# A DRAIN on GpSimd in each pass of the loop over expert tiles

## What is computed

```python
def _moe2_ref(x, w_gate, w_local, w1, w2):
    logits = np.einsum('bsd,de->bse', x, w_gate)
    local_gate = 1.0 / (1.0 + np.exp(-np.einsum('bsd,de->bse', x, w_local).squeeze(-1)))
    for b in range(B):
        prev_e = -1
        for s in range(S):
            fresh_e = int(np.argmax(logits[b, s]))
            if s == 0 or local_gate[b, s] < 0.5:
                e = fresh_e
            else:
                e = prev_e if prev_e >= 0 else fresh_e
            prev_e = e
            ...                                  # p: softmax of logits[b, s]
            h = np.maximum(x[b, s] @ w1[e], 0.0)
            out[b, s] = p[e] * (h @ w2[e])
```

## Time and profile before

| | |
|---|---|
| median of 3 runs | 627.32 us (628.27, 627.32, 627.22) |
| profiled execution, its own time | 628.33 us |
| its span, first to last instruction | 626.3 us |
| mean granted TensorE clock | 0.995 |
| busy: PE, DVE, ACT, POOL | 97%, 66%, 51%, 28% of the span |

### The profile page before, as it was taken

How to read it: one execution, slowest core, us unless ns; L and a number is a source line. 1 busy time by engine, 2 the same in 40 slices (tenths; PEclk the granted TensorE clock), 3 DMA queues, 4 the chain that set the end, 5 groups by cost and what they waited for, 6 DMA issues and landing times.

```text
span 626.3 us, 14701 instructions
## 1 busy us (share of the span) xinstructions
PE 607.7 (97%) x4483; PEld 504.6 (81%) x4484; DVE 410.8 (66%) x1164; ACT 321.3 (51%) x698; POOL 176.2 (28%) x241
## 2 busy tenths in 40 slices
PE   7999999999999999999999999999999999999994
PEld 6778888888788888889979877788788888888883
DVE  3767779745779697786979959948626336372621
ACT  5767779667515714631544853647516226351610
POOL 4545545600000000000000231675723412552240
PEclk9999999999999999999999999999999999999998
DMA  8987786002210010000004751787825414672000
GB/s 302 374 269 249 265 278 220 18 2 85 74 62 0 1 50 18 0 33 35 0 32 155 247 223 57 282 304 258 326 82 174 167 39 131 214 245 93 12 29 3
DMA packets 32935, 84.66 MB, mean 135 GB/s; under 512 B 4602, under 2 KB 7418, under 8 KB 32896
## 3 DMA queue, kind: packets, MB, share of 16 engines
q1 hardware_dynamic: 26816, 70.03, 32.0%
q0 software_dynamic: 3200, 8.92, 4.2%
q10 hardware_dynamic: 2880, 5.24, 2.6%
HBM read 76.04 MB, written 9.70 MB: 137 GB/s over the span
## 4 chain that ended last, share of the span: by engine, by line
PE 82%; DVE 8%; issue 3%; ACT 2%; POOL 2%; DMA 1%; POOLq 0%; DVEq 0%; ACTq 0%
PE banks L884 21%; PE banks L886 20%; PE banks L885 20%; PE banks L755 3%; PE banks L1074 3%; PE banks L822 2%; DVE we_lo L1526 2%; PE banks L831 2%; PE banks L785 2%; PE banks L769 1%; PE banks L993 1%; PE banks L799 1%; PE banks L795 1%; DMA xg<-x_rows,rows_in 1%; PE banks L846 1%
## 5 line engine op out<-in xcount | busy, mean ns | idle before, releaser
L1493 DVE CUSTOM_DVE_ANT_0 product<-x,xT 128x512 f32<-128x512 f32 x120 | 77.9, 688 | 0.5 <-DMA xT<-in_w 0.3
L1790 ACT ACTIVATE prob<-neg,negmax 128x160 f32<-128x160 f32 (+1 forms) x136 | 59.1, 436 | 30.3 <-DVE negmax L1204 20.6
L1768 DVE TENSOR_SCALAR hid<-banks 128x512 f32<-128x512 f32 x34 | 23.5, 691 | 72.4 <-PE banks L886 71.2
L1900 ACT ACTIVATE k_sum<-banks 128x512 f32<-128x512 f32 (+2 forms) x40 | 21.3, 534 | 90.9 <-PE banks L886 86.3
L884 PE MATMUL banks<-we_hi,hid_hi 128*128 (+1 forms) x160 | 66.4, 415 | 0.2 <-DVE hid_lo L1601 0.2
L884 PE MATMUL banks<-we_hi,xg_hi 128*128 (+1 forms) x160 | 64.6, 404 | 0.6 <-issue 0.6
L686 POOL MEMSET xg<- 128x1024 f32 x1 | 1.0, 952 | 220.9 <-ACT k_raw L1893 220.9
L886 PE MATMUL banks<-we_hi,xg_lo 128*128 (+1 forms) x160 | 62.6, 391 | 0.0
L885 PE MATMUL banks<-we_lo,hid_hi 128*128 (+1 forms) x160 | 62.6, 391 | 0.0
L886 PE MATMUL banks<-we_hi,hid_lo 128*128 (+1 forms) x160 | 62.6, 391 | 0.0
L885 PE MATMUL banks<-we_lo,xg_hi 128*128 (+1 forms) x160 | 62.4, 390 | 0.0
(11 more groups left out here) (295 smaller groups left out, 1486.0 us busy)
## 6 DMA issues: line engine op xcount, KB each, us to landing
xT<-in_w_e SPq DMA_DIRECT2D x36, 512.0 KB, 4.3
raw_end<-in_w_e SPq DMA_DIRECT2D x36, 512.0 KB, 5.0
qk<-in_qk_t SPq DMA_DIRECT2D x32, 448.0 KB, 6.2
vw<-in_v_t SPq DMA_DIRECT2D x32, 256.0 KB, 5.1
w_raw<-in_w_mix ACTq DMA_DIRECT2D x20, 256.0 KB, 4.2
x_rows<-x SPq DMA_DIRECT2D x17, 256.0 KB, 2.0
xT<-in_w SPq DMA_DIRECT2D x8, 256.0 KB, 3.3
vz<-in_v_z SPq DMA_DIRECT2D x8, 128.0 KB, 3.5
```

What stands on the lines that cost most here:

```text
L1493: dve.tensor_tensor_reduce(product[:, k % 2, :], x2[:, t, :], w9(e), 1.0, 0.0, ALU.mult, ALU.add, dot[:, t % 2, e:e + 1]).then_inc(dotted, 1)
L1768: dve.tensor_scalar(hid[:, D * h:D * (h + 1)], ps_h[:, h, :], 0.0, None, ALU.max).then_inc(hid_ready, 1)
L1790: act.activation(prob[:, t % 2, c], neg[:, c], ACT.Exp, scale=-1.0, bias=negmax[:, t % 2, k:k + 1], accum_out=rsum[:, t % 2, k:k + 1]).the ...
L1900: act.activation(k_sum[:, f % 2, 0:w], ps_k[:, f % 2, 0:w], ACT.Relu).then_inc(k_copied, 1)
```

## The change

GpSimd gets one instruction more in each of the two passes of its loop: a DRAIN, behind the low parts (or behind the jump over them) and ahead of the register arithmetic and the wait on `y_stored`. A DRAIN keeps the sequencer from going on until what it has handed to its engine is done.

```diff
                         with pool.If(after > 0):
                             last_parts(after, bass.ds(after % 2, 1))
+                        pool.drain()

                         pool.wait_ge(y_stored[b], 16 * (k + 1 - b))
                         pool.sem_inc(stepped, 1)
                         scatter(i, b)
```

## The result

The change made the kernel faster: 623.42 us against 627.22 (medians of 9 runs each), a ratio of 0.9946 with a 95% interval of 0.9930 to 0.9961. By the ratio that is 3.4 us, between 2.4 and 4.4 (the two medians lie 3.8 us apart); the forecast was no change. The time lies outside the forecast's range.

A forecast was written before the change was run, and what follows sets the result against it. The prediction took TensorE, 97% busy, to bound the kernel; three kinds of passes at 0 us each, from the median 627.32 with a tenth for a leak, gave 627.4 us; range from 626.7 less 0.1 to 628.6.

The forecast's parts named there:

- What bounds the kernel: Whole loop: runs at TensorE's own speed, 97% busy; GpSimd touches it only at one gather, a 0.4 us wait.
- The cost of a DRAIN: Each pass of GpSimd's loop: the copy of row numbers begins 0.36 us later, with ends of 0 and 1.0 us.
- Passes whose store waits for the output: Passes where GpSimd waits for ScalarE's output, the last included: the 0.36 us comes out of that wait, 0 us.
- The early gather: Pass at 420.66 us: the next gather may be up to 5.37 us late before the low parts notice, 0 us.
- The pass on the chain: Low parts at 432.33 us: the later copy still ends at 440.34, held by VectorE's instruction, so the gather stays, 0 us.
- A: Loop's gather on the chain: a DRAIN over about 2 us makes it late, 628.5 up to 629.7 us; chance 0.03.
- B: Store at 441.33 us: shifted, it can't write descriptors while VectorE works; gather 3.7 us later, 631.0 us; chance 0.02.
- C: TensorE's waits in the loop: a gather meets less DMA traffic, giving back at most 0.6 us, 626.7 us; chance 0.02.
- D: GpSimd's loop: the DRAIN does nothing, engine empty or sequencer let go at once, 627.3 us; chance 0.05.
- E: Copy behind the low parts: not held by VectorE, so the 0.36 us is not absorbed, 627.7 us; chance 0.06.

The follow-up runs named there:

- the two versions: The change, a DRAIN in every pass, 623.42 us against 627.22; and the kernel before with one DRAIN in the last pass alone, 622.95 us against 626.95.

## Why the prediction was wrong, step by step

**What bounds the kernel: half right.** The loop runs at TensorE's speed, and the loop did not change. But the kernel does not end with the loop. The chain of waits ended with the last store, at 619.61 + 0.98 = 620.59, and the span is 626.3: 5.7 us behind it that I never asked about. The chain is followed back from the last instruction that an engine itself executed; the closing DRAIN is the sequencer's and comes behind it, so it is neither in the chain nor in a busy share. It stood in the trace of before all the same, 3343 ns beside 7 to 17 on other engines; the sentence "the trace has no DRAIN in the loop" was true and looked in the wrong place.

**The cost of a DRAIN, 0.36 us between 0 and 1.0: wrong.** Those in the loop took 1.2 to 6.3 us, counted from where the sequencer reached them. Only behind the low parts was the gap, 0.57 us, near the estimate: the DRAIN ended 0.25 us behind them (at 438.47), and the copy began 0.32 us later. Behind a gather it was 2.5 to 3.2 us, and behind a store alone 2.1 and 2.2, since the DRAIN waits for the landing. I bounded the price by GpSimd's wait for its own copy, and took a DMA to be over when its issue was.

**Passes whose store waits for the output, 0 us: right in result,** with 2.1 to 2.9 us taken out of each wait instead of 0.36. The 10 waits of 65.3 us became 6 of 33.9, where the prediction had them shrink "hardly at all". In the same step stands the sentence that fails: "The end of the kernel doesn't move". The last store was not moved by the DRAINs; what came behind it was.

**The early gather, 0 us: right, with little to spare.** From the gather at 420.66 to the next at 425.90 it was 5.24 us, after it was 428.16 - 419.69 = 8.47. The idle time ahead of the low parts, named as the room, shrank from 5.37 to 1.27 us. The DRAIN ahead of the loop shows what happens without such room: 3.7 us of TensorE.

**The pass on the chain, 0 us: right, mechanism and numbers.** The copy came 0.57 us late and ended 439.34 - 438.22 = 1.12 us behind the low parts, before 440.34 - 439.20 = 1.14. Both times that is 0.04 to 0.05 us behind VectorE's low part, which after ended at 439.30:

```profile
437.93 1.37 DVE L1527 TENSOR_TENSOR we_lo<-xT,we_hi 128x1024 f32 x1
```

The gather did not move (12.39 against 12.41 us). TensorE's wait of 0.4 us for these rows is absent after; with the gather where it was against the low parts, that belongs to how the two streams lay in this execution, and no experiment was made for it.

**The rivals.** A (a dear DRAIN makes a gather late) did not occur in the change, but it did with the DRAIN ahead of the loop: 6.4 us between the two stores, and 4.8 us above the median in one execution. B did not occur: the store at 440.35 took 1.02 us. C held the failing premise in one sentence: "A DRAIN can only hold GpSimd back." Its bound, 0.6 us, came from TensorE's waits in the loop alone. D was wrong, and E did not occur: the copy was held by VectorE. No rival had the right mechanism, that a DRAIN settles something which a later DRAIN at the end would have to.

**The size.** 0.0825 us x 39 = 3.2 us off the end, none put on elsewhere: 627.3 - 3.2 = 624.1, a ratio of 0.995; measured 623.4 and 623.0 in the two versions, with 0.995 inside both intervals of the ratio. The step that failed is the sentence "The end of the kernel doesn't move: 0 us", and with it the sum, which had no term for what lies between the last work and the end of the span. The runs put -3.2 us in its place.

## What to carry to other kernels

Read what stands between the last busy instruction and the end of the span, sequencer rows included, before any sum; here it was 5.7 us and held the whole effect. This kernel's GpSimd issues 40 DMAs and pays 3.3 us for them in its closing DRAIN; one DRAIN of one's own in the last stretch where GpSimd waits anyway takes that off the end. Look for the same in any kernel whose GpSimd issues many. Put it where the sequencer has some 3 us and more to give, and not ahead of a gather that TensorE is about to need: there the wait cost 3.3 us and the fallen clock as much again.

## What the hardware showed that was not expected

- With nothing left to wait for, a DRAIN on GpSimd takes 0.04 us + 0.0825 us for each DMA that GpSimd issued since its last DRAIN, indirect or direct, 6 or 128 rows, over eight counts from 0 to 59. Idle time does not settle it (10.4 us of idle ahead of the last store in the kernel before), nor does a semaphore wait for the landing.
- It also waits for the landing of DMAs still under way: 3.50 us beside a gather of 3.3, 3.30 beside one of 3.1. With 39 to settle and a store begun 1.6 us before, it took 3.26 us, what the line alone gives: the settling and the wait overlap. They don't always do so in full: the loop's first DRAIN, with nine to settle, took 3.91 us beside a gather that landed in 3.5, and so ended some 0.4 us behind the landing. No run tells why.
- What is settled (descriptors taken back, or other bookkeeping) no run showed; only what it is proportional to.
- A small copy on GpSimd that began while VectorE's instruction with two operands in SBUF ran ended with it: 0.55 us for the one at 438.79, 1.19 us for the earlier one at 439.15 of before, 0.04 and 0.05 us behind VectorE's.
- TensorE's granted clock fell to 0.51 during an idle time of 3.7 us, and stayed there for 6.8 us, most of them busy.
